# Expert stage's first x: the low half moves from GpSimd to VectorE, and GpSimd clears the accumulator first

## The reference, cut to what matters

```python
def _moe2_ref(x, expert_emb, tau, w1, w2):
    xn = x / (np.linalg.norm(x, axis=-1, keepdims=True) + 1e-06)
    en = expert_emb / (np.linalg.norm(expert_emb, axis=-1, keepdims=True) + 1e-06)
    logits = xn @ en.T / tau
    expert_idx = np.argmax(logits, axis=1)
    probs = np.exp(logits - logits.max(-1, keepdims=True))
    probs /= probs.sum(-1, keepdims=True) + 1e-09
    gate_w = probs[np.arange(N), expert_idx]
    for e in range(E):
        mask = expert_idx == e
        if not mask.any():
            continue
        h = np.maximum(x[mask] @ w1[e], 0.0)
        out[mask] = gate_w[mask, None] * (h @ w2[e])
```

## Time and profile before

| what | us |
|---|---|
| median of 3 runs (lowest, highest) | 768.75 (768.74, 770.08) |
| profiled execution, its own time | 767.32 |
| its span, first to last instruction | 765.2 |
| PE busy | 722.6 (94%) |
| DVE busy | 407.1 (53%) |
| POOL busy | 118.6 (16%) |

### The profile page before, as it was taken

The page is one execution under the profiler, slowest core; times in us unless marked ns, Lnnn a source line. Parts: engine busy times, 40 slices in busy tenths (PEclk is TensorE's granted clock), DMA queues, the critical chain, the costliest instruction groups (busy, mean ns, idle before and its releaser), DMA issues. The chain is left out here.

```text
span 765.2 us, 12834 instructions
## 1 busy us (share of the span) xinstructions
PE 722.6 (94%) x4947; PEld 607.1 (79%) x4948; DVE 407.1 (53%) x687; ACT 311.4 (41%) x545; POOL 118.6 (16%) x149
## 2 busy tenths in 40 slices
PE   5899999999999999999999999997199999999995
PEld 4688888888888888888888888885089999998995
DVE  6878786755566556655566554543644222223321
ACT  3577665434454445444454446444232212112120
POOL 6300012222221122222222100000520000000000
PEclk9999999999999999999999999999589999999998
DMA  8883122011121111011010001001520120202011
GB/s 151 210 221 74 29 53 64 12 30 33 32 73 32 33 32 56 19 32 32 11 43 2 1 1 42 1 0 43 194 97 21 63 83 1 83 1 82 20 62 41
DMA packets 88317, 40.36 MB, mean 53 GB/s; under 512 B 77113, under 2 KB 84929, under 8 KB 88257
## 3 DMA queue, kind: packets, MB, share of 16 engines
q1 hardware_dynamic: 86400, 34.61, 17.9%
q10 hardware_dynamic: 1856, 4.93, 1.7%
HBM read 30.10 MB, written 9.44 MB: 52 GB/s over the span
## 5 line engine op out<-in xcount | busy, mean ns | idle before, releaser
L946 PE MATMUL x_ps<-g_p,wout_hi 128*128 128x512 f32 x576 | 182.5, 398 | 0.2 <-DVE g_p L726 0.2
L964 PE MATMUL h_ps<-x0T,win_hi 128*128 128x512 f32 x576 | 178.3, 391 | 1.9 <-DVE x0T L654 1.9
L509 ACT ACTIVATE above<-h_ps,minus_one 128x512 f32<-128x512 f32 x96 | 66.0, 688 | 170.0 <-DVE mid L739 169.5
L964 PEld LDWEIGHTS h_ps<-x0T,win_hi 128*128 128x128 f32 x576 | 107.5, 188 | 24.7 <-DVE x0T L654 2.2
L946 PEld LDWEIGHTS x_ps<-g_p,wout_hi 128*128 128x128 f32 x576 | 104.6, 188 | 22.2 <-issue 1.4
L1503 PE MATMUL ch_ps<-x_p,w_p 128*128 128x512 f32 x432 | 109.1, 400 | 12.1 <-DVE w_p L1569 12.1
L739 DVE TENSOR_SCALAR mid<-h_ps 128x512 f32<-128x512 f32 x96 | 66.2, 690 | 98.6 <-PE h_ps L964 98.1
L946 PE MATMUL x_ps<-g_p,wout_lo 128*128 128x512 f32 x288 | 112.6, 391 | 0.0
L964 PE MATMUL h_ps<-x0T,win_lo 128*128 128x512 f32 x288 | 112.1, 389 | 0.0
L748 DVE TENSOR_TENSOR mid<-mid,above 128x512 f32<-128x512 f32 x96 | 70.8, 738 | 70.8 <-ACT mid L510 70.7
L1492 PE MATMUL cy_ps<-w_p,h_p 128*128 128x384 f32 x576 | 107.7, 336 | 0.0
(11 more groups left out here) (214 smaller groups left out, 621.4 us busy)
## 6 DMA issues: line engine op xcount, KB each, us to landing
xr<-xT_scratch SPq DMA_DIRECT2D x8, 768.0 KB, 5.0
rkv<-in_v SPq DMA_DIRECT2D x24, 192.0 KB, 2.9
xT_scratch<-xbuf ACTq DMA_DIRECT2D x6, 768.0 KB, 3.4
out<-acc SPq DMA_DIRECT2D x12, 384.0 KB, 2.4
rkv<-in_r SPq DMA_DIRECT2D x20, 192.0 KB, 3.5
rkv<-in_k SPq DMA_DIRECT2D x20, 192.0 KB, 3.7
win_raw<-in_moe_w_in SPq DMA_DIRECT2D x48, 64.0 KB, 3.3
wout_raw<-in_moe_w_out SPq DMA_DIRECT2D x4, 768.0 KB, 6.8
```

The lines of the kernel that those rows point to most:

```text
L509: raises(act.activation(above[:, f % 2], h_ps[f % 2][:, :], ACT.Relu, bias=minus_one[:, :]), "over")
L946: last = pe.matmul(x_ps[kk][:, :], (wout_hi, wout_lo)[a][:, f, cols], g_p[:, at % NG, b], start=(f == 0 and n == 0), stop=(f == NF1 - 1 an ...
L964: last = pe.matmul(h_ps[f % 2][:, :], (win_hi, win_lo)[a][:, f // QF, kk, cols], x0T[:, c % 2, b, kk], start=(kk == 0 and n == 0), stop=(k ...
```

## The change

POOL no longer makes the low half of x chunk 0. DVE does, in three subtractions of 128x512, between the scaled difference (which sets off ACT's exponential) and the sum of the exponentials. POOL's memset of `acc` moves from the end of its program to the place where the subtractions stood, ahead of the wait for `counts_ready`. On DVE the difference to the largest logit moves ahead of the norms.

```diff
@@ POOL
-                for kk in range(KD):
-                    wait(pool, "x_hi", 0, kk + 1)
-                    raises(pool.tensor_tensor(x_p[:, 0, 1, kk], xr[:, 0, kk], x_p[:, 0, 0, kk].bitcast(FP32),
-                                              ALU.subtract), "x_lo")
-
+                pool.memset(acc[:, :, :], 0.0).then_inc(cleared, 1)
                 last_step = [0]
...
                 pool.tensor_copy(last_i[:, :, :], cum[:, :, :]).then_inc(last_ready, 1)
-                pool.memset(acc[:, :, :], 0.0).then_inc(cleared, 1)
@@ DVE
-                dve.wait_ge(rooted, 1)
-                norm_from_root(dve, link, logits[:, :, E], root[:, :], tmp[:, :], inv[:, :])
-
-                link(dve.tensor_tensor(diff[:, :, :], lg, over_e(top), ALU.subtract))
-                dve.tensor_tensor(diff[:, :, :], diff[:, :, :], over_e(inv), ALU.mult).then_inc(scaled, 1)
...
+                link(dve.tensor_tensor(diff[:, :, :], lg, over_e(top), ALU.subtract))
+                dve.wait_ge(rooted, 1)
+                norm_from_root(dve, link, logits[:, :, E], root[:, :], tmp[:, :], inv[:, :])
+                dve.tensor_tensor(diff[:, :, :], diff[:, :, :], over_e(inv), ALU.mult).then_inc(scaled, 1)
+                for kk in range(KD):
+                    x_lo(0, 0, kk)
                 dve.wait_ge(exped, 1)
```

## The result

The changed kernel takes 772.73 us (median of 5 runs, 771.9 to 773.18), the kernel before 768.87 (median of 5, 768.74 to 770.08): ratio 1.0046 with a 95% interval of 1.0031 to 1.0061. It is slower: by 3.9 us between the medians, by 3.5 us by the ratio, whose interval is 2.4 to 4.7 us. The forecast was 772.6, slower.

The account below looks back on a forecast made before the run. PE is busy 94% of the span, but its first expert matmul waits on a serial DVE chain. There -2.52 + 1.47 + 4.68 (hold) + 0.3 gave +3.9 us on the 768.75 median: 772.6, range 767.2 to 774.2.

Parts of the forecast that it names:

- The hold: DVE's cast of `has` waits for the end of POOL's memset, now first: +4.68 us, chance 0.66.
- What the change takes away: POOL's subtractions no longer hold DVE's cast of `order` and two 128x24 sums, L97 and L98: -2.52 us.
- What it adds: Three subtractions on DVE, 1.88 us, less the 0.41 wait for ACT's exponential: +1.47 us.
- Contention behind the hold: DVE's small instructions after the hold run beside POOL's sums, eleven at 0.025 each: +0.3 us, between 0 and 1.4.
- The sum: Stretch to the first expert matmul, with the hold: -1.05 + 4.68 + 0.3 = +3.9 us.
- What is late next: DMAs of the expert weights: 1.2 us of slack before DVE's low half, staying with the hold, so they cost nothing.
- Memset holds nothing: Rival: the cast of `has` goes past POOL's memset unheld; -1.05 us, 767.7 us; chance 0.27.
- Holds two-input instructions as well: Rival: POOL's memset also holds DVE's two-input instructions, first L1532; +6.6 us, 775.4 us; chance 0.04.
- The subtractions are not what held DVE: Rival: DVE's long instructions stay long, -2.52 falls away; without a memset hold +1.5, 770.2 us; chance 0.03, shared with swallowed moves.

Follow-up runs that it names:

- last run: Against the kernel before: three subtractions on DVE behind the gates, POOL's memset behind its sums and waiting for DVE's last scalar operation ahead of the gates; 766.57 us, ratio 0.9972.
- half-and-half run: Changed kernel with only half of POOL's memset of `acc` first and the other half behind its sums; ratio 1.0034 to the kernel before.

## Why the prediction was right, point by point

**The hold.** This term decided the sign, and no row of before had it. Forecast 4.68 us on the cast of `has`, measured 4.83 - 0.18 = 4.65. What was an inference from the held one-input cast and the free two-input subtraction is now shown directly: the same numbers in two forms, 0.20 and 4.83 us. The Trainium skill ("SBUF — State Buffer", "Who interferes with whom") says of copies, casts and scalar operations in a 2-port mode that a GpSimd instruction blocks them, and of two-input instructions that only one that reads SBUF does. The holds by the memset (`has` 4.83, `active` 4.46, L95 2.23, L99 7.59) and the free two-input instructions under it (0.36, 0.20, 0.15) agree with that.

**What the change takes away.** Forecast -2.52. The cast of `order` 1.02 to 0.16, L97 811 to 201 ns, L98 1169 to 184 ns: 0.86 + 0.61 + 0.99 = -2.46.

**What it adds.** Forecast 1.88 for three subtractions, measured 1.89, with no wait for the exponential behind them. From the end of the scaled difference to the end of the gates it was 1.84 (548.75 to 550.59) and is 3.03 (553.33 to 556.36): +1.19, forecast +1.47. The term was 0.28 too large: 0.17 of it is at the seams, where the first subtraction starts 0.08 ahead of the difference's end and the sum 0.09 ahead of the last one's, and 0.12 is in the gates' product, below.

**Contention behind the hold.** Forecast +0.3, and this term was wrong in size: it is about nothing. The gates' product, 483 ns before, is even back at 0.36, with POOL's sums over by then (its last ends at 552.68); that is in the +1.19 already. L95 is 0.05 longer than before. With the other three terms as measured, 4.65 - 2.46 + 1.19 = 3.38, this one comes out at 3.30 - 3.38 = -0.08.

**The sum.** It said +3.9, and the stretch grew by 3.30: 0.38 of the difference is the contention and 0.28 the term before it; the rest nearly cancels. The ratio says 3.5. That the forecast of the median fits to a tenth (772.6 and 772.73) is luck; the right sign and the right size to within 0.6 us are not. The first expert matmul was forecast at 557.4 and stands at 559.21, 2.45 of it from the stage's later start.

**What is late next.** The slack of the weights was forecast at 1.2 us; the high half of the first piece ends at 557.03 and DVE takes it at 558.11, so 1.1. This slack is what the last run uses up.

**The rivals.** "Memset holds nothing" falls by the cast of 4.83. "Holds two-input instructions as well" falls by L1527, which takes its 0.36 under the memset. "The subtractions are not what held DVE" falls by L97 and L98. In one point the prediction's list of what the memset could hold was too short: it had the three casts. Scalar operations are held as well (`active` 4.46, L95 2.23), so with `has` alone rewritten the stretch stayed at 18.06, and the cast of one element, `n_listed`, is not held.

**What I had not seen.** The forecast did not ask what kept the memset harmless in its old place, and priced the two edits as separate. In fact the subtractions on POOL were what pushed the memset behind DVE's last scalar operation: it began at 551.00 when the last, L1573, had started at 549.55. Take them off POOL and the memset is harmful in its old place, too, by more (21.41 against 18.14).

## What to carry to other kernels

When an engine loses work, look at what then starts earlier on it and at what it will meet: the memset in its old place in the program was the worst of all. A long GpSimd memset is dangerous to VectorE by the kind of what runs beside it, so put it beside reductions and two-input instructions and give it a wait that keeps it there (stretch 13.72). Cutting it with a wait between the pieces is second best (15.54); pieces alone don't help (18.57). This holds for a memset, which only writes: the subtractions of GpSimd, which read, held two-input instructions too (L97 and L98). And independent work belongs directly ahead of VectorE's register loads: three subtractions there hid 1.8 us and, with the 0.41 of ACT's exponential back, saved 1.37.

## What the runs showed of the hardware that I had not expected

Back-to-back GpSimd instructions kept a waiting VectorE cast out over their seams: 8.49 us through a memset and three subtractions, 5.26 us through the rest of 12 memsets of 0.7 each. A semaphore wait between the pieces let it in within one piece (0.63 to 0.77). In the kernel before, though, two instructions got in at the seams of three subtractions that also followed each other closely. POOL's second and third, and DVE's L97 and L98:

```profile
544.87 2.49 POOL L1392 TENSOR_TENSOR x_p<-xr,x_p 128x512 fp32r<-128x512 f32 x2
```

```profile
545.39 0.81 DVE L97 TENSOR_TENSOR tmp<-tmp,logits 128x24 f32<-128x24 f32 x1
546.23 1.17 DVE L98 TENSOR_TENSOR tmp<-tmp,root 128x24 f32<-128x24 f32 x1
```

The cast of `order` ended at 544.93, with the first subtraction over at 544.92 and the second begun at 544.87. L97 ended at 546.20, with the second over at 546.14 and the third begun at 546.11. So it is neither the form nor the size of the held instruction by itself, since a cast of 8 numbers and a two-input instruction of 128x24 both got in. Both had started to wait during a subtraction, where the ones kept out had met a memset, or, like L99 in the run with the memset last and in the half-and-half run, a small cast with a memset right behind it. Whether that is the difference no run here separates; it stays open.

A cast of one element was never held (0.14 us under a memset in two kernels), one of 8 elements was (0.75 under a waiting piece, 1.02 in the earlier trace rows under a subtraction). The reciprocals of 128x24 keep their 0.30 throughout, in the earlier trace rows under a subtraction of POOL.

VectorE's queue loads registers while its engine works off instructions that it already has: 1.8 us went under 1.9 us of subtractions.
